# Five normalising instructions per batch moved from GpSimd to VectorE in a RoPE attention and gated MLP kernel

## The reference

```python
q_rot, k_rot = rotate(q), rotate(k)                       # RoPE
scores = (1/sqrt(D)) * q_rot @ k_rot^T                    # 576 x 576 per head
attn = exp(scores - max(scores, axis=-1))
attn = attn / (sum(attn, axis=-1) + 1e-9)
x = (attn @ v) with the heads side by side                # 4 x 576 x 512, fp32
h = relu(x @ w_in)                                        # 512 -> 1024
y = (h * sigmoid(conv3(h))) @ w_out                       # 1024 -> 512
```

## Time and profile before

| what | value |
|---|---|
| three runs, us | 559.77, 560.39, 563.61; median 560.39 |
| the profiled execution's own time, us | 559.77 |
| its span, first to last instruction, us | 558.0 |
| mean granted TensorE clock | 0.941 |
| busy: PE, DVE, ACT, POOL | 447.1, 411.2, 279.5, 213.6 us |

### The profile page before, as it was taken

How to read it: one execution, slowest core, us unless ns; L and a number is a source line. 1 busy time by engine, 2 the same in 40 slices (tenths; PEclk the granted TensorE clock), 3 DMA queues, 4 the chain that set the end, 5 groups by cost and what they waited for, 6 DMA issues and landing times.

```text
span 558.0 us, 16269 instructions
## 1 busy us (share of the span) xinstructions
PE 447.1 (80%) x6784; PEld 399.9 (72%) x6784; DVE 411.2 (74%) x776; ACT 279.5 (50%) x655; POOL 213.6 (38%) x297
## 2 busy tenths in 40 slices
PE   0036668877999698877999799887999699897996
PEld 0035556767999586666999577677999477687996
DVE  6977477776994879876994988786994987945531
ACT  1233555435675644535575554435675544535552
POOL 4324477631433445421333454421433443521321
PEclk9999989788999889999999698798999897999999
DMA  6798421124658102233757110233757111200011
GB/s 212 214 268 241 173 88 38 51 88 119 189 163 244 53 13 80 87 114 93 208 160 237 43 54 38 86 106 103 209 161 224 53 47 45 87 4 1 2 43 43
DMA packets 24362, 62.47 MB, mean 112 GB/s; under 512 B 3296, under 2 KB 7392, under 8 KB 21984
## 3 DMA queue, kind: packets, MB, share of 16 engines
q1 hardware_dynamic: 24288, 61.43, 36.1%
HBM read 42.55 MB, written 4.72 MB: 85 GB/s over the span
## 4 chain that ended last, share of the span: by engine, by line
PE 54%; DVE 19%; issue 9%; DMA 6%; ACT 5%; POOL 5%; SPq 1%; POOLq 0%; DVEq 0%; ACTq 0%
PE banks L366 14%; DVE neg_max L610 6%; PE banks L338 6%; PE banks L398 5%; PE banks L400 5%; PE banks L399 5%; DVE turned L639 5%; PE banks L382 4%; PE banks L384 4%; PE banks L383 4%; PE banks L339 4%; DVE conv L650 3%; DVE x_lo L644 2%; DMA KL<-Q 2%; DMA wi_raw<-w_in_dram 1%
## 5 line engine op out<-in xcount | busy, mean ns | idle before, releaser
L475 ACT ACTIVATE P<-banks,neg_max 128x576 f32<-128x576 f32 x144 | 106.5, 740 | 127.1 <-DVE neg_max L610 126.0
L763 POOL TENSOR_SCALAR P<-P,recip 128x576 f32<-128x576 f32 x144 | 106.2, 748 | 131.3 <-DVE recip L627 130.4
L338 PE MATMUL banks<-K,Q 128*128 128x288 f32 x256 | 94.1, 379 | 71.2 <-ACT P L475 38.0
L610 DVE TENSOR_REDUCE neg_max<-banks 128x1 f32<-128x576 f32 x144 | 106.8, 742 | 47.4 <-PE banks L339 36.5
L338 PEld LDWEIGHTS banks<-K,Q 128*128 128x128 f32 x256 | 56.2, 219 | 97.6 <-issue 53.1
L767 POOL TENSOR_TENSOR u_lo<-u,u_hi 128x288 fp32r<-128x288 f32 x64 | 59.5, 930 | 171.9 <-ACT u_hi L508 171.9
L639 DVE STREAM_TRANSPOSE turned<-P 128x576 f32<-128x576 f32 x144 | 109.2, 761 | 4.1 <-PE banks L366 3.7
L366 PE MATMUL banks<-turned,V 32*64 32x128 f32 (+1 forms) x4608 | 101.4, 303 | 8.4 <-issue 5.7
L650 DVE SCALAR_TENSOR_TENSOR conv<-banks,taps,conv 128x288 f32<-128x288 f32 x128 | 65.5, 512 | 42.6 <-ACT conv L497 42.4
L366 PEld LDWEIGHTS banks<-turned,V 32*64 32x64 f32 x4608 | 81.5, 136 | 21.2 <-issue 17.8
L382 PE MATMUL banks<-x_hi,wi_hi 128*128 128x290 f32 x256 | 79.7, 311 | 15.6 <-DVE u L658 11.8
(11 more groups left out here) (49 smaller groups left out, 607.5 us busy)
## 6 DMA issues: line engine op xcount, KB each, us to landing
V<-v_rows_dram SPq DMA_DIRECT2D x16, 1152.0 KB, 5.5
xc<-qk_dram SPq DMA_DIRECT2D x28, 288.0 KB, 3.1
xs<-qk_swapped_dram SPq DMA_DIRECT2D x28, 288.0 KB, 4.5
KL<-Q SPq DMA_DIRECT2D x32, 144.0 KB, 4.4
Q<-K SPq DMA_DIRECT2D x32, 144.0 KB, 4.2
K<-K SPq DMA_DIRECT2D x32, 144.0 KB, 3.6
y_dram<-y_sb SPq DMA_DIRECT2D x8, 576.0 KB, 3.3
wi_raw<-w_in_dram SPq DMA_DIRECT2D x1, 2048.0 KB, 8.1
```

The source lines that it names most:

```text
L338: nc.tensor.matmul(out, Q[:, h, qc], K[:, h, cols], start=True, stop=False)
L475: nc.scalar.activation(dst, src, ACT.Exp, bias=neg_max[:, c:c + 1], scale=1.0, accum_out=row_sum[:, c:c + 1]).then_inc(exps, 1)
L610: nc.vector.tensor_reduce(out=neg_max[:, c:c + 1], in_=banks[:, 2 * (t % 2):2 * (t % 2) + 2, 0:HALF], axis=AX.XY, op=ALU.max, negate=True) ...
L763: nc.gpsimd.tensor_scalar(p, p, recip[:, c:c + 1], 1.0, ALU.mult, ALU.mult).then_inc(normed, 1)
```

## The change

The tiles of the first three groups of each batch (pair 0, tiles 0 to 4) are normalised by DVE in `first_maxima`, each group right behind its reciprocals or one maximum later, and no longer by POOL. They are counted by a semaphore of their own, `first_normed`; POOL's tiles keep `normed`, with the counts shifted.

```diff
-        normed = sem("normed")
+        normed, first_normed = sem("normed"), sem("first_normed")
...
         def tile_normed(b, pair, i):
-            return normed, b * N_SCORES + tiles_before(pair, i) + 1
+            n, ahead = tiles_before(pair, i) + 1, FULL + 1
+            if n <= ahead:
+                return first_normed, b * ahead + n
+            return normed, b * (N_SCORES - ahead) + (n - ahead)
...
                 add_eps(b, 0, 0)
                 reciprocals(b, 0, 0)
                 max_tile(b, 0, 3)
+                normalise_group(b, 0)
                 turn(b, 0)
                 max_tile(b, 0, 4)
                 add_eps(b, 0, 1)
                 reciprocals(b, 0, 1)
+                normalise_group(b, 1)
                 turn(b, 1)
                 max_tile(b, 0, 5)
                 add_eps(b, 0, 2)
                 reciprocals(b, 0, 2)
+                normalise_group(b, 2)
+
+            def normalise_group(b, k):
+                dve.wait_ge(recips, b * N_GROUPS + (k + 1))
+                for i in range(*GROUPS[k]):
+                    p = p_tile(0, i)
+                    nc.vector.tensor_scalar(p, p, recip[:, i:i + 1], None, ALU.mult).then_inc(first_normed, 1)
...
             def attention(b, first):
                 for pair in range(PAIRS):
                     for k, (a, e) in enumerate(GROUPS):
-                        if pair > 0 or k > 2:
-                            add_eps(b, pair, k)
+                        if pair == 0 and k < 3:
+                            continue
+                        add_eps(b, pair, k)
                         for i in range(a, e):
                             normalise(b, pair, i)
```

## The result

The changed kernel took 566.48 us (median of 11 runs, 564.88 to 570.83), the kernel before 563.3 us in the runs beside it (559.07 to 569.19). The ratio is 1.0086, with a 95% interval of 1.006 to 1.011: 0.86% slower, some 4.8 us of 561 (3.4 to 6.2 by the interval). The forecast was 0.6% slower (3.5 us), at 563.9 us. That absolute number started from the median of three runs, 560.39; eleven runs put the same kernel at 563.3, so ratios say more here than microseconds.

The account below looks back on a forecast made before the run. It took DVE's full queue at the head of each batch as the bound. Batches 0 to 3 added 0 + 1.12 + 1.28 + 1.12 = 3.5 us to 560.4, giving 563.9 us; range 560.5 to 567.5.

Parts of the forecast that it names:

- What bounds the head: Start of each batch: from tile 4's maximum DVE's queue is the bound, busy 5.45 us of 5.60 in batch 1.
- What goes: POOL loses 3.7 us of normalising per batch; the relief was counted at nothing.
- What one added instruction costs: Each multiplication added to DVE takes 0.45 us and moves the next by 0.37; upper end 0.76 and 0.69.
- Group 0: Tiles 0 and 1, batches 1 to 3: two instructions add 0.74 us, covered by DVE's wait for PE.
- group 1: Tiles 2 and 3: two multiplications wait for the reciprocals, so tile 1's transpose starts 0.85 us late.
- group 2: Tile 4: one multiplication adds 0.43 us, so tile 6's maximum is 1.28 us late.
- What passes on: From tile 7's maximum on, the delay stays: 1.12 us in batches 1 and 3 after 0.16 slack, 1.28 in batch 2.
- Batch 0: First batch: a delay of 1.3 us ends in DVE's 6.78 us gap for the weights' DMA; cost nothing.
- One column per step: Rival: the DVE multiplication costs what the transpose costs; sum 6.7 us, 567.1 us, 1.2% slower; chance 0.12.
- the handover: Rival: POOL's answer is on the path; gain at most 1.2 us against 3.5, giving 562.7; no separate chance given.
- The clock did not give the loss back: Rival: PE's slow chunks with V vanish in later batches, returning 3.5 us, 560.4; chance 0.13, shared with the head hiding it.
- the rival of more clock loss: Rival: one or two more slow PE chunks with V, 565.6 to 567.3 us; chance 0.06.

Follow-up runs that it names:

- e2: Changed kernel, but only tiles 2 to 4 of each batch normalised on DVE, tiles 0 and 1 back on POOL; ratio 1.0107 to the kernel before.
- e1: Changed kernel, but only tiles 0 and 1 of each batch normalised on DVE, the rest back on POOL; ratio 1.0014 to the kernel before.
- e3: Changed kernel, but the five tiles normalised on DVE in batch 0 only, on POOL in batches 1 to 3; ratio 1.0013 to the kernel before.
- e6: Changed kernel with each normalising DVE instruction cut in two of 288 columns; ratio 1.0113 to the kernel before.
- e9: Changed kernel with unused PE matmuls, 6 and 5 ahead of tiles 6 and 7, then 2 or 3 up to tile 13; ratio 0.9948 to before.
- e7: Kernel before with unused PE matmuls, 6 and 5 ahead of tiles 6 and 7, then 2 or 3 up to tile 13; ratio 0.9871.
- e5: Kernel before with 2 or 3 unused PE matmuls ahead of the scores of each of tiles 6 to 13; ratio 0.9885.
- e8: Changed kernel with ten unused POOL instructions beside DVE's multiplications of tiles 2 to 4 in batches 1 to 3; ratio 1.0164 to before.

## Why the prediction was right or wrong

**What bounds the head: right.** The full DVE queue from tile 4 on was the place of the loss (e2); in DVE's wait for PE ahead of it and in the wait for the weights no cost is seen (e1, e3).

**What goes: right.** POOL's relief bought nothing; the 0.3 us of wait in batch 0 vanished in the weights' gap.

**What one added instruction costs: right in kind, too small.** The small cast pointed to two columns per step, and e6 confirms them. The fixed part was the error. It was taken from instructions that read PSUM, 154 ns, and is 214 for this one. Why is open: the 64-column cast, from SBUF to SBUF as well, takes 184 ns in all, less than that fixed part alone. The instruction took 0.516 us, not 0.448, and moved the next by 0.43, not 0.37. Over three instructions in a head that is 0.2 us. The estimate worked out from the Trainium skill (VectorE: DVE Perf Modes), 457 ns, was short in the same way (the page has its 151 cycles from an fp32 `tensor_tensor`); the measurement decides. Its rule of two results a cycle was right, and the nearest row in size, the transpose, was the wrong guide.

**Group 0, group 1, group 2.** Group 0: covered, as forecast. Group 1: tile 5 is 1.00 us later, forecast 0.85. Group 2: tile 6 is 1.51 us later, forecast 1.28; the difference of 0.23 is the three steps of 0.06 and the wait for the reciprocals.

**What passes on: the step that failed.** The forecast let 0.16 us of slack at tile 7 absorb a part and passed on 1.12 us in batches 1 and 3, with PE's clock as it was before (in batch 2 the low clock was taken over, and there the whole 1.28). At a full clock the runs show 1.29 to 1.30 (e9 against e7), which is this step with the larger instruction: 1.51 less 0.2 of slack. But in the changed kernel 1.70, 1.51 and 1.68 passed on. In batches 1 and 3 the slack was not there, and more than the delay of tile 6 passed on, since PE waited longer and its clock fell at tile 7 in place of tile 11. The prediction had named that direction among the rivals ("a longer head makes PE idler, which speaks for more such places") and priced it only at the products with V.

The sum fell short by 1.37 us, 4.89 against 3.52, in two equal parts. 0.69 us are the sizes of groups 1 and 2, 0.23 in each of the three heads; in batch 2 that is the whole miss (1.51 against 1.28), and taking over the low clock there was right. The other 0.68 us are the failed step in batches 1 and 3: with the true sizes it would have passed on 1.35 us in each, and 1.70 and 1.68 were measured.

**Batch 0: right that it costs nothing to be seen, not in the size.** The gap for the weights shrank to 6.23 us in the changed kernel and 6.09 in e3, not to 5.5: in batch 0 DVE had 0.50 us of wait for PE ahead of tile 6, which took up a part, and the weights came 0.4 and 0.3 us later behind tile 4 than before.

**The rivals.** One column per step did not come true (0.516 us), the handover neither. The clock did not give the loss back; it added to it, in the head itself. The changed kernel's profile also has one more chunk with V at 2.36 us, in batch 1, as the rival of more clock loss had it, but e3, which is unchanged in batch 1, has one there too. The clock is worth more than the whole change: e7's filling takes 1.3%.

**The signs.** Tile 4 to tile 7 took 5.63 us in batches 1 and 3 (5.2 forecast for batch 1) and 5.43 in batch 2 (5.4 forecast), which points at the same step. The span from the head of batch 1 to that of batch 2 grew by 4.3 us, not by 1.1 to 1.3: 1.70 in the head, 2.1 in the rest of the attention, where the clock differed. The sign that the difference would lie in PE's clock came true in part, for 1.01 of 4.89 us.

**The chances.** Within 1% had 0.80, and the ratio, 1.0086, is within 1%. But its interval reaches over 1%, and does not hold 1, so the loss is measured: 0.86 where 0.6 was forecast, with slower by over 1% at 0.17. The median of 566.48 us lies in the range of 560.5 to 567.5, but little follows from it: of the 2.6 us over the forecast's 563.9, none is left once the kernel before is taken at 563.3 and not at 560.4. The profiled execution, forecast at 563.3 us, took 568.65 and lies outside.

## What to carry to other kernels

In this kernel work moved to a nearly full queue cost its issue distance (the time from its start to the next one's) wherever the queue had no gap, and nothing where it waited; so go through the timeline instruction by instruction and place it in the waits (e1 is such a change, and free). When a stretch becomes longer for one engine, ask what the idler PE's clock does in it, and price that at the same place. Before weighing a small gain in a stretch at half clock, try a few unused matmuls in PE's waits: here they were worth more than what was being moved.

## What the runs showed of the hardware that was not expected

- Unused matmuls make the kernel faster. Where PE had idled and its granted clock stood at 0.65 to 0.81 over the head (a mix of its levels of 1.2 and 2.4 GHz), 20 matmuls more in each head (e5) or 26 (e7) held it at 1.00 (2.4 GHz) and took 1.3 us off each: 0.9885 and 0.9871 for the kernel before.
- DVE's multiplication of 128x576 fp32 in SBUF by a column per partition runs at 0.52 ns per column with 214 ns fixed, where the two instructions that read PSUM showed 154. The next instruction starts 0.08 to 0.09 us before its end (0.43 us after its start), as behind others.
- Beside POOL instructions that read and write SBUF it takes longer, in e8 0.84 us in place of 0.52. The Trainium skill (GPSIMD Engine Reference, Key points) says that POOL shares its SBUF interfaces with DVE in a two-port mode; this case agrees and adds the price, 0.65 us for three instructions.
